# Attention in split precision: the mixed tile's low product of k as one matmul for both heads

## The reference

```
q, k, v: (batch 4, heads 8, seq 576, head_dim 64), float32
scores = 1/sqrt(64) * q @ k^T
x      = log1p(|i - j|) / log1p(max(i, 1))
scores = scores + (relu(x * w1 + b1) @ w2)[i, j, head]     # hidden size 32
attn   = exp(scores - max) ;  attn = attn / (sum(attn) + 1e-9)
out    = attn @ v                       # tokens (4*576, 8*64) for the next stages
```

## Time and profile before

| what | value |
|---|---|
| median of three runs | 1020.74 us |
| profiled execution, its own time | 1022.32 us |
| its span from first to last instruction | 1020.5 us |
| mean granted TensorE clock | 0.991 |
| attention, first to last score matmul | 57.4 to 281.2 us |
| TensorE busy in the span | 985.1 us |
| VectorE busy in the span | 774.1 us |

### The profile page before, as it was taken

One profiled execution on the slowest core, in us unless ns is written; L12 is line 12 of the kernel. 1 busy time (PEld: TensorE's weight loads), 2 busy tenths in 40 slices (PEclk: granted clock), 3 DMA queues, 4 the chain that ended last, 5 costly groups with the idle time before them and its releaser, 6 DMA issues.

```text
span 1020.5 us, 27753 instructions
## 1 busy us (share of the span) xinstructions
PE 985.1 (97%) x10129; PEld 858.0 (84%) x10130; DVE 774.1 (76%) x1197; ACT 419.7 (41%) x830; POOL 202.9 (20%) x190
## 2 busy tenths in 40 slices
PE   6888999999989999999999999999999999999997
PEld 2357888888878999999999999888888888888996
DVE  8998999999948477565564799787767787777674
ACT  7975666666626356353443433311221122112211
POOL 1035655556403122221220000010010001000101
PEclk9979999999999999999999999999999999999999
DMA  4883867677316746325121700030110011000100
GB/s 153 303 293 148 268 206 279 191 256 257 117 40 238 267 145 217 129 95 178 46 93 64 267 22 1 1 96 1 42 41 0 0 31 42 1 1 1 42 1 31
DMA packets 66559, 117.44 MB, mean 115 GB/s; under 512 B 27120, under 2 KB 36384, under 8 KB 64464
## 3 DMA queue, kind: packets, MB, share of 16 engines
q1 hardware_dynamic: 62480, 103.45, 30.0%
q0 software_dynamic: 4032, 13.37, 3.8%
HBM read 91.41 MB, written 25.40 MB: 114 GB/s over the span
## 4 chain that ended last, share of the span: by engine, by line
PE 68%; DVE 1%; ACT 0%; DMA 0%; issue 0%; POOL 0%; POOLq 0%; DVEq 0%
PE psum L1821 28%; PE psum L1829 14%; PE psum L1306 11%; PE psum L1315 11%; PE psum L1292 1%; PE psum L899 1%; DVE f_eg L1774 0%; PE psum L1355 0%; DMA e_xin<-x_tokens,r_idx 0%; PE psum L919 0%; DVE f_alo L1761 0%; ACT f_ahi L1731 0%; POOL e_xin L1262 0%; PE psum L600 0%; ACT e_xin L1371 0%
## 5 line engine op out<-in xcount | busy, mean ns | idle before, releaser
L1774 DVE RECIPROCAL f_eg<-f_eg 128x512 f32<-128x512 f32 (+1 forms) x60 | 181.6, 3026 | 0.0
L1740 ACT ACTIVATE f_eg<-psum 128x512 f32<-128x512 f32 (+1 forms) x60 | 33.4, 556 | 316.9 <-PE psum L1821 316.9
L1821 PE MATMUL psum<-f_x,f_ghi 128*128 128x384 f32 (+2 forms) x480 | 138.0, 368 | 0.4 <-DVE f_x L1633 0.4
L1821 PE MATMUL psum<-f_x,f_vhi 128*128 128x384 f32 (+2 forms) x480 | 137.4, 367 | 0.0
L694 ACT ACTIVATE a_pr<-a_sc,a_nmax 128x576 f32<-128x576 f32 x144 | 110.9, 770 | 63.9 <-DVE a_nmax L633 63.4
L633 DVE CUSTOM_DVE_ANT_0 a_sc<-psum,a_bias 128x576 f32<-128x576 f32 x144 | 104.2, 744 | 15.6 <-issue 5.8
L1707 POOL DMA_INDIRECT out<-f_ob,f_cols x18 | 17.8, 987 | 458.1 <-ACT f_ob L1724 318.9
L463 PE MATMUL psum<-a_khi,a_qs 128*128 128x288 f32 x320 | 100.7, 334 | 5.0 <-DVE a_nmax L633 3.9
L587 PE MATMUL psum<-a_pt,a_v 32*64 32x160 f32 (+1 forms) x4608 | 101.0, 296 | 4.2 <-issue 4.1
L644 DVE STREAM_TRANSPOSE a_pt<-a_pr 128x576 f32<-128x576 f32 x144 | 104.1, 757 | 0.0
L1821 PEld LDWEIGHTS psum<-f_x,f_ghi 128*128 128x128 f32 x480 | 89.2, 188 | 13.5 <-DVE f_x L1633 0.6
(11 more groups left out here) (239 smaller groups left out, 2100.2 us busy)
## 6 DMA issues: line engine op xcount, KB each, us to landing
a_v<-v SPq DMA_DIRECT2D x16, 1152.0 KB, 5.7
e_raw<-ew SPq DMA_DIRECT2D x16, 1024.0 KB, 5.8
bias_ihj<-b_res SPq DMA_DIRECT2D x36, 288.0 KB, 2.8
a_bias<-bias_ihj SPq DMA_DIRECT2D x16, 576.0 KB, 6.6
a_qraw<-q SPq DMA_DIRECT2D x15, 576.0 KB, 4.3
a_kraw<-k SPq DMA_DIRECT2D x15, 576.0 KB, 5.3
xn_t<-e_yn SPq DMA_DIRECT2D x8, 576.0 KB, 3.1
x_tokens<-a_xp SPq DMA_DIRECT2D x64, 64.0 KB, 3.4
```

Of the source, the lines that this page charges most:

```text
L1740: e.activation(self.eg[:, k % 2, 0:w], self.g_ps[k % 2][:, 0:w], ACT.Exp, scale=-1.0).then_inc(self.s_e, 1)
L1774: e.reciprocal(x, x).then_inc(self.s_c, 1)
L1821: mm = e.matmul(acc[:, 0:width], a, b, start=(q == 0 and i == 0), stop=(q == KD - 1 and i == 2))
```

## The change

The product of q with the low part of k is done for both heads at once in the mixed tile. Two new tiles hold its operands:

- `a_kmix`: partitions 0 to 63 hold `a_klo` of head 0, partitions 64 to 127 `a_klo` of head 1. Since `a_klo` has each head in other columns, transfers bring them together: two DMAs of 64 partitions by 576 elements, issued by SyncE at the top of each pair, behind a wait for GpSimd's split of that pair.
- `a_qmix`: a block diagonal of the unsplit q, 64 rows of head 0 by 64 columns and 64 rows of head 1 by 64 columns, zeros elsewhere. ScalarE writes the two blocks with two ACTIVATE copies of 64 by 64, for pair p + 1 in step 0 of pair p; GpSimd sets the zeros once.

The mixed tile's four matmuls per half become three. TensorE waits ahead of them for `a_qmix` and for the landing of both transfers. SyncE waits for `a_qmix` (which also reads the raw q) ahead of the load that overwrites the raw q.

```
 def scores(e, p, u, uses, s, h):
...
-        parts = [(0, BLK), (1, S)] if s == MIX else [(h, 704 * h + P * s)]
+        if s == MIX:
+            e.wait_ge(s_qm, sem.at(s_qm, p + 1))
+            sem.apart(e, p)
+            e.wait_ge(s_km[u], sem.at(s_km[u], uses * 32 + 32))
+            sem.apart(e, uses)
+            ops = [(qs[:, u, BLK:BLK + P], khi, 0), (qs[:, u, S:S + P], khi, S), (qmix[:, u, :], kmix, 0)]
+        else:
+            c = 704 * h + P * s
+            ops = [(qs[:, u, c:c + P], khi, S * h), (qs[:, u, c:c + P], klo, S * h)]
         for half in range(2):
-            ops = [(a, c, k) for a, c in parts for k in (khi, klo)]
-            for i, (a, c, k) in enumerate(ops):
-                mm = e.matmul(s_ps[:, h, half, 0:HALF], qs[:, u, c:c + P],
-                              k[:, u, a * S + half * HALF:a * S + (half + 1) * HALF],
+            for i, (q, k, at) in enumerate(ops):
+                mm = e.matmul(s_ps[:, h, half, 0:HALF], q, k[:, u, at + half * HALF:at + (half + 1) * HALF],
                               start=(i == 0), stop=(i == len(ops) - 1))
...
+        def mix_k(p, u):
+            split_done(e, p)
+            for h in range(2):
+                rows = slice(64 * h, 64 * h + 64)
+                e.dma_start(kmix[rows, u, :].bitcast(f32), klo[rows, u, S * h:S * h + S].bitcast(f32)).then_inc(s_km[u], 16)
+
         def pair(p, u, uses):
+            mix_k(p, u)
...
             def next_qk():
-                split_done(e, p)
+                e.wait_ge(s_qm, sem.at(s_qm, p + 1))
+                sem.apart(e, p)
                 load_qk(e, (p + 2) % NPAIR, u)
...
+        def mix_q(p, u, uses):
...
+            e.wait_ge(s_q[u], sem.at(s_q[u], uses * 16 + 16 + 16 * u))
+            sem.apart(e, uses)
+            e.activation(qmix[0:64, u, 0:64], qraw[0:64, u, 0, BLK:S], ACT.Copy)
+            e.activation(qmix[64:P, u, 64:P], qraw[64:P, u, 1, 0:64], ACT.Copy).then_inc(s_qm, 1)
...
                 if exists(np_) and ns != MIX:
                     exps(np_, nu, nuses, ns, 1)
+                if s == 0 and exists(p + 1):
+                    mix_q(p + 1, 1 - u, uses + u)
```

More of the change, by code:

```diff
@@ L304, in front_stages @@
     kraw = arena.at("a_kraw", [P, 2, 2 * S], arena.LATE)
+    kmix = arena.at("a_kmix", [P, 2, S], arena.LATE + 16 * S, f32r)
+    qmix = arena.at("a_qmix", [P, 2, P], arena.LATE + 24 * S, f32r)
     vv = arena.at("a_v", [P, 2, NK, P], arena.FRONT)
@@ L313, in front_stages @@
     s_k0 = sem("a_k0hi")
+    s_qm, s_km = sem("a_qmix"), [sem("a_kmix0"), sem("a_kmix1")]
     s_sp, s_kk, s_qh, s_ql, s_low = sem("a_sp"), sem("a_kk"), sem("a_qh"), sem("a_ql"), sem("a_low")
@@ L342, in set_constants @@
                 .then_inc(s_init, 1)
-        e.wait_ge(s_init, sem.at(s_init, 5))
+        e.memset(qmix[:, :, :].bitcast(f32), 0.0).then_inc(s_init, 1)
+        e.wait_ge(s_init, sem.at(s_init, 6))
     def first_high(e):
@@ L708, in normal @@
             x.then_inc(s_xf, 1)
+        def mix_q(p, u, uses):
+            if isinstance(p, int) and p < 2:
+                e.wait_ge(s_init, sem.at(s_init, 6))
+            e.wait_ge(s_q[u], sem.at(s_q[u], uses * 16 + 16 + 16 * u))
+            sem.apart(e, uses)
+            e.activation(qmix[0:64, u, 0:64], qraw[0:64, u, 0, BLK:S], ACT.Copy)
+            e.activation(qmix[64:P, u, 64:P], qraw[64:P, u, 1, 0:64], ACT.Copy).then_inc(s_qm, 1)
         def keep_out(p):
@@ L736, in scalar @@
             exps(0, 0, 0, 0, h)
+        mix_q(0, 0, 0)
         each_pair(e, pair)
```

## The result

| | median | lowest to highest | runs | profiled execution | its span |
|---|---|---|---|---|---|
| before | 1020.78 us | 1019.93 to 1023.17 | 5 | 1022.32 | 1020.5 |
| changed | 1036.48 us | 1033.21 to 1039.80 | 5 | 1033.21 | 1031.4 |

The changed kernel is slower: its time is 1.0157 of before's, with a 95% interval of 1.0141 to 1.0173, or 15.7 us more. The prediction said 1023.8 in a range up to 1034, so the time lies outside the range, on the side forecast. The traces show 10.9 us of the difference (1031.4 − 1020.5): the profiled execution of the changed kernel is its fastest, 3.3 us under the median, and the one of before lies 1.5 above its own. The other 4.8 us lie in executions without a profile.

What follows compares the result with a forecast made beforehand. TensorE was taken to set the pace, VectorE within a microsecond of it. Matmuls −4.0, waits +0.3, copies behind bias pairs +5.1 and pair 0 +1.7 gave +3.1 us on the 1020.7 median: 1023.8 us, range 1017.5 to 1034.

Steps and rivals of the forecast that it cites:

- The queue runs ahead of the matmuls: TensorE ahead of the mixed tile: two added waits and two counting instructions cost 0.02 us a pair, 0.3 in all.
- The saving: Mixed tile on TensorE: two of eight matmuls go, 0.266 us a pair, 4.0 us less over pairs 1 to 15.
- The copy in a plain pair: Nine plain pairs: the second half of `a_kmix` lands 0.4 and 0.1 us ahead of the mixed tile, so costs nothing.
- Behind the bias pairs: Pairs 4, 8 and 12: bias issues hold up the stores, so `a_kmix` lands 1.7 us late each, 5.1 us in all.
- The bound of 3.6 us: Longest landing allowed for `a_kmix`, from 64-partition stores; behind bias pairs it would cost 3 × 3.2 us.
- Pair 0: Start: copies follow two bias issues and land late for the mixed tile, 1.7 us lost, 1.3 least, 3.2 most.
- ScalarE's copies: Two 64 × 64 copies, 0.44 us a pair, covered by ScalarE's idle time; nothing counted, up to 6 us if uncovered.
- The traffic and the later loads of q and k: 288 KB more per pair fit beside a DMA share of 0.60, q and k load 1.1 us later; nothing counted.
- The rival on that stall: Pair 2: TensorE's 2.20 us stall may not come with the changed code; 3.7 us go, 1020.1 us; chance 0.13.
- Late everywhere: Landing takes 3.0 us: nine plain pairs lose 0.5 to 0.8 us each, bias pairs 0.9 more; 1032.3 us; chance 0.24.
- Short landing: `a_kmix` lands in 1.9 us, giving 1022.8 us, or 1021.6 at 1.6 us: no measurable change; chance 0.15.
- all hidden: Copies issued earlier or landing well under 1 us everywhere, only the matmul saving left: 1017.0 us; chance 0.08.

## Why the prediction was wrong

The direction came out, and so did the mechanism of its largest term, the late copies behind the bias pairs. Two terms that were put at nearly nothing weren't (+4.1 us for the waits, +4.6 for the copies that nobody reads), and together they are more of the miss than the mis-sized landing. Point by point:

- **"The queue runs ahead of the matmuls", two waits for 0.02 us.** This step failed. The two waits with their counting instructions cost 0.20 us a pair with their conditions long met (the waits alone: +4.1 us in all, 3.0 of it by the pairs), and 0.39 us a tile in the changed kernel. I had set the bound at 0.2 from a single distance and then chosen near nothing, on an assumption that no row showed.
- **The saving, 0.266 us a pair.** Mis-sized: 0.195 us, 3.1 us in all, as the kernel with six matmuls showed. A quarter of it is lost, and with it VectorE's waiting for TensorE: its 0.9 us of idle time, which I took for room, was room for less than 0.266. Together with the waits nothing is left: −3.1 and +4.1, where the sum had −4.0 and +0.3.
- **The copy in a plain pair, hidden by 0.1 to 0.4 us.** About right in place, and worth little. The second copy goes out 6.04 us behind the v load (201.34 + 0.57 − 195.87), predicted 5.68, and TensorE starts 2.59 us after it, predicted 2.2. The wait named in the trace is 0.16 us, but with the copies a pair earlier the distance is the same. So it was hidden, though behind instructions that the sum had at nearly nothing.
- **Behind the bias pairs, 1.7 us each.** The mechanism was right and the place of the issue too: stores done 6.90 us behind the v load, predicted 6.89. The landing was mis-sized: TensorE starts 2.56 us after the second issue in pair 8 (187.97 to 190.53), 3.54 in pair 4 (129.26 to 132.80) and 3.05 in pair 12, where I had 2.2. That is 2.6 us in all. I argued that v and the stores "have nearly drained"; the DMA share of 1.02 says that they hadn't. The three pairs lost 7.17 us, net of saving, where the forecast had 4.4. The bound of 3.6 us held.
- **Pair 0, 1.7 us.** TensorE waited 1.88 us, and the next tile came 1.55 later than before. About right. That pair 1's stall would grow by 1.14 us behind it, no term had.
- **ScalarE's copies, nothing.** Right (1.0003).
- **The traffic and the later loads of q and k, nothing.** This failed, and no rival named it in this form. The copies alone cost 4.6 us; of the 3.4 that the profile shows, 3.1 are there by pair 2's v load. The rival on that stall had it the wrong way round: it got longer, 2.62 us. In the four profiles with all copies behind the stores it is 2.62 to 3.02 us, in the five without copies or with pair 0's only 1.92 to 2.20.
- **Rivals.** "Late everywhere" (1032.3) came nearest in time, yet not in its mechanism: nine plain pairs were to lose 0.5 to 0.8 us to the landing, and came out 0.1 longer each, net of the saving. "Short landing" fell with the landing of 2.3 us at least and 2.4 in the median. Two of these sums had slips that change nothing in the outcome: "late everywhere" left out pair 0, which would be 0.9 us later too, and the 1017.0 of "all hidden" lies below the range that was to hold it.

Landings of `a_kmix` from issue, as the trace gives them:

```profile
DMA to landing us min/median/max: 2.3/2.4/10.1
```

The Trainium skill (DMA: Bandwidth & Descriptors, Anatomy of one DMA) gives 2.34 us by its fit. The fit is stated for transfers that GpSimd issues, which the prediction left out, and these went out on SyncE; the trace agrees all the same, 2.3 at least and 2.4 in the median. What the same section says of HBM as the heaviest target I had taken to speak for less than the 1.9 us of the stores, and no copy into SBUF was as short. The comparison was uneven, too: those stores carry 16 KB each, a copy 144 KB.

Do the parts make the whole? By the kernels that had one part each: −3.1 for the matmuls, +4.1 for the waits, +4.6 for the traffic, +0.6 for ScalarE (not told from nothing) are +6.2. To these come the waits for `a_kmix`, 9.6 us in one profile and 8.1 in the other: 15.8 and 14.3, against 15.7 and 13.8 measured. That it closes to 0.1 us is partly luck. The waits come from single profiles, the first of which shows 10.9 of the 15.7 us only, and the waiting instructions took 0.39 us a tile in the changed kernel, not the 0.20 that the +4.1 stands for. Read from the other side, the earlier copies gave 13.0 us back by the medians and 10.2 in the profiles (1031.4 less 1021.2). Of these 10.2, 7.9 are waits for `a_kmix` (9.6 to 1.7) and 2.0 the stall of pair 2, 0.64 us instead of 2.62. That stall varied from one kernel to the next (2.00 us with the moved wait), and whether the place of the copies sets it was not tried by itself.

## What to carry to other kernels

A wait in a loop isn't free on an engine that runs dense, even if its condition has long been met: where TensorE sets the pace, price each added wait with its counting at 0.1 to 0.2 us, as measured here, and weigh it against the matmul that it buys, or put it where the engine stands still anyway. In the pair outside the loop, with fixed numbers and no counting, the same waits cost nothing. For a new transfer, ask what is still in flight at its issue, not only when the queue comes to it: behind the bias loads the same copy took up to 1 us longer, and moving the issues alone made it worse. Allow for the clock as well: idle time of TensorE can be followed by a stretch at the lower one. And a hand-off in the steady state can be all right while the pairs at the start, where everything loads at once, pay for it.

## What the runs showed of the hardware

- Two waits with their counting instructions, met long before, put the next matmul 0.27 us behind the last instead of 0.13, lengthened the block by 0.20, and in the changed kernel stood for a distance of 0.44 to 0.46 us and 0.39 more in the block. One such wait: a distance of 0.18 to 0.23 us in the plain pairs. Two waits for fixed numbers, without counting (pair 15): 0.13 us, nothing.
- An SBUF to SBUF copy of 64 partitions and 144 KB landed in 2.3 us at least and in 2.4 in the median, behind bias loads in 2.5 to 3.4, and with the bias issued first in 3.0 to 4.6; a store of 64 partitions and 16 KB to HBM took 1.9 and 2.8 us.
- Issuing on SyncE isn't of fixed length: two stores took 3.54, 2.32 and 1.61 us to issue instead of 1.3, in the stretches behind the v load of three bias pairs.
- TensorE's stall in pair 2, for which the trace names no one, was 1.9 to 2.2 us without the copies and 2.6 to 3.0 with all of them behind the stores. The profile's page lists transfers of instructions, a queue of its own (29 packets, 0.48 MB). That such a transfer comes later with more data in flight would explain it; no run here shows it.
- After idle time of TensorE the granted clock fell in some executions and not in others: 0.57 over the 4 us behind a wait of 2.00 us, 0.50 behind one of 3.32, and 1.00 behind one of 2.61. Behind the stall of pair 2 it was 0.83 from 95 to 105 us in the profile of before.
